# Turns of a constant on TensorE before the first scores, and a part of q moved from GpSimd to VectorE

## The reference

```
scores = q @ k.T / 8
thresh = max(scores) - tau
scores = where(scores >= thresh, scores, -1e9)
attn   = exp(scores - max(scores)); attn = attn / (sum(attn) + 1e-9)
out    = attn @ v
```

## Time and profile before

| | us |
|---|---|
| three runs | 1113.57, 1113.32, 1110.95 |
| median | 1113.32 |
| the profiled execution | 1109.99 |
| its span (first to last instruction) | 1108.2 |

### The profile page before, as it was taken

The page is one execution under the profiler, slowest core; times in us unless marked ns, Lnnn a source line. Parts: engine busy times, 40 slices in busy tenths (PEclk is TensorE's granted clock), DMA queues, the critical chain, the costliest instruction groups (busy, mean ns, idle before and its releaser), DMA issues.

```text
span 1108.2 us, 18294 instructions
## 1 busy us (share of the span) xinstructions
PE 1053.6 (95%) x6504; PEld 988.9 (89%) x6504; DVE 833.9 (75%) x1544; ACT 610.0 (55%) x1121; POOL 513.1 (46%) x594
## 2 busy tenths in 40 slices
PE   4888899999999999998999999989999998999998
PEld 4766799999999999998999999978898988899897
DVE  4999978787878888767885847888584799867561
ACT  4888786868676776644452516445251544534240
POOL 3567755554545564564561405456050546514050
PEclk9999999999999999999999999989999999999999
DMA  4447453437234543462224041432203143330302
GB/s 120 119 135 189 126 136 112 114 94 174 88 110 112 141 112 99 113 167 81 87 87 137 1 134 58 129 97 80 92 1 106 29 124 105 96 124 29 114 1 86
DMA packets 117227, 112.44 MB, mean 101 GB/s; under 512 B 28672, under 2 KB 100496, under 8 KB 117136
## 3 DMA queue, kind: packets, MB, share of 16 engines
q1 hardware_dynamic: 116832, 110.97, 35.6%
q10 hardware_dynamic: 304, 0.30, 0.1%
HBM read 78.12 MB, written 33.10 MB: 100 GB/s over the span
## 4 chain that ended last, share of the span: by engine, by line
PE 79%; DVE 12%; issue 4%; ACT 3%; DMA 1%; POOL 1%; SPq 1%; ACTq 0%; POOLq 0%; DVEq 0%
PE score L785 11%; PE score L824 10%; PE mm L785 8%; PE score L706 8%; PE mm L744 7%; PE tr L721 6%; PE mm L751 6%; PE mm L735 6%; PE tr L824 5%; PE tr L785 4%; PE score L822 3%; DVE prob L927 2%; PE tr L822 2%; PE mm L822 2%; DVE neg_max L919 1%
## 5 line engine op out<-in xcount | busy, mean ns | idle before, releaser
L1593 POOL TENSOR_TENSOR gd_lo<-act_ring,gd_hi 128x384 fp32r<-128x384 f32 x144 | 155.2, 1098 | 289.0 <-ACT gd_hi L1345 287.3
L1236 ACT ACTIVATE pt_hi<-tr 128x640 fp32r<-128x640 f32 x144 | 101.7, 706 | 98.3 <-PE tr L721 97.8
L919 DVE TENSOR_REDUCE neg_max<-score 128x1 f32<-128x576 f32 x144 | 108.3, 752 | 27.4 <-PE score L706 24.5
L945 DVE TENSOR_TENSOR pt_lo<-tr,pt_hi 128x640 fp32r<-128x640 f32 x144 | 118.3, 821 | 10.1 <-ACT pt_hi L1236 9.2
L706 PE MATMUL score<-k_hi,q_sp 128*128 128x288 f32 x320 | 98.3, 323 | 28.8 <-DVE prob L927 20.0
L1536 POOL TENSOR_SCALAR thresh<-neg_max,tau_abs 128x1 f32<-128x1 f32 x144 | 41.7, 290 | 179.3 <-DVE neg_max L919 178.7
L927 DVE SCALAR_TENSOR_TENSOR prob<-score,thresh,prob 128x576 f32<-128x576 f32 x144 | 116.3, 808 | 0.0
L721 PE MATMUL tr<-ident,prob 128*128 128x128 f32 x720 | 105.5, 278 | 8.0 <-issue 5.9
L1231 ACT ACTIVATE prob<-score,neg_max 128x576 f32<-128x576 f32 x144 | 106.5, 739 | 7.8 <-DVE neg_max L919 7.5
L721 PEld LDWEIGHTS tr<-ident,prob 128*128 128x128 f32 x720 | 83.5, 143 | 18.5 <-issue 17.7
L706 PEld LDWEIGHTS score<-k_hi,q_sp 128*128 128x128 f32 x320 | 62.3, 195 | 40.3 <-DVE prob L927 30.2
(11 more groups left out here) (172 smaller groups left out, 3259.1 us busy)
## 6 DMA issues: line engine op xcount, KB each, us to landing
pair_raw<-x_t_scratch SPq DMA_DIRECT2D x72, 192.0 KB, 3.2
q_raw<-in_qT SPq DMA_DIRECT2D x64, 144.0 KB, 2.8
k_raw<-in_kT SPq DMA_DIRECT2D x62, 144.0 KB, 2.9
unit_raw<-in_w_in SPq DMA_DIRECT2D x48, 128.0 KB, 2.5
unit_raw<-in_w_out SPq DMA_DIRECT2D x48, 128.0 KB, 2.3
o_parts_scratch<-o_t SPq DMA_DIRECT2D x32, 160.0 KB, 1.8
x_t_scratch<-x_raw SPq DMA_DIRECT2D x8, 576.0 KB, 3.1
part_t_scratch<-y_out SPq DMA_DIRECT2D x8, 576.0 KB, 3.3
```

Of the source, the lines that this page charges most:

```text
L919: dve.tensor_reduce(neg_max[:, r:r + 1], score[:, g % 2, :, 0:HALF], AX.XY, ALU.max, negate=True).then_inc(max_done, 1)
L945: dve.tensor_tensor(pt_place(pt_lo, x), turned_place(x), pt_place(pt_hi, x), ALU.subtract).then_inc(pt_lo_done, 1)
L1236: act.activation(pt_place(pt_hi, x), turned_place(x), ACT.Copy).then_inc(pt_hi_done, 1)
L1593: pool.tensor_tensor(gd_lo[:, u, c, :], act_ring[:, g % 3, :], gd_hi[:, u, c, :], ALU.subtract).then_inc(g_lo_done, 1)
```

## The change

TensorE runs 32 transposes of `ident` against itself into the bank that the real turns use later, before the first scores. Tile 0 waits for k's high part where it waited for k's low part, and its second matmul waits for the low part. VectorE, not GpSimd, makes the low part of q's first 256 columns, between k's high part and k's low part.

```
@@ tensor: scores(g)
                 if g == 0:
                     pe.wait_ge(first_q_lo_done, 1)
-                    pe.wait_ge(first_k_lo_done, 1)
+                    pe.wait_ge(first_k_hi_done, 1)
...
                     for e, (side, col, k_part) in enumerate(parts):
+                        if g == 0 and half == 0 and e == 1:
+                            pe.wait_ge(first_k_lo_done, 1)
                         m = pe.matmul(score[:, g % 2, half, 0:HALF], q_sp[:, col:col + P],
@@ tensor: start
             pe.wait_ge(consts_done, 8)
+
+            for _ in range(32):
+                pe.transpose(turned_p[:, 0:P], ident[:, :], ident[:, :])
             scores(0)
@@ vector: start
             dve.tensor_copy(k_hi[:, 0, :], k_raw[:, 0, :]).then_inc(first_k_hi_done, 1)
+            begin = slice(0, 2 * P)
+            dve.wait_ge(first_q_scaled, 1)
+            dve.tensor_tensor(q_sp[:, begin], q_raw[:, 0, begin], q_sp[:, begin], ALU.subtract).then_inc(first_q_lo_done, 1)
             dve.wait_ge(first_k_hi_done, 1)
@@ gpsimd: start
-            begin, rest = slice(0, 2 * P), slice(2 * P, S)
-            pool.wait_ge(first_q_scaled, 1)
-            pool.tensor_tensor(q_sp[:, begin], q_raw[:, 0, begin], q_sp[:, begin], ALU.subtract).then_inc(first_q_lo_done, 1)
+            rest = slice(2 * P, S)
             pool.wait_ge(q_scaled, 1)
```

## The result

| | kernel before | changed kernel |
|---|---|---|
| median of 13 runs, us | 1111.17 | 1107.98 |
| lowest and highest, us | 1109.35, 1113.59 | 1106.83, 1112.08 |
| the profiled execution, us | 1109.99 | 1107.62 |

The ratio is 0.9972, with a 95% interval of 0.9961 to 0.9983: 3.1 us faster, between 1.9 and 4.3. That is 0.28%, just inside the 0.3% named above. The median of before came out 2.1 us lower over 13 runs than over the first three. The prediction's range, 1108.0 to 1114.2, was counted from 1113.3: 5.3 us less to 0.9 more. The change of 3.1 us lies inside it, while 1107.98 as a bare time lies at its very edge.

What follows compares the result with a forecast made beforehand. TensorE's work and its waits (79% of the span) were taken to bound the kernel. An earlier first maximum, 0.7, plus one faster tile, 0.5, made 1.2, taken as 1.3 us: 1113.3 to 1112.0 us, range 1108.0 to 1114.2.

Steps and rivals of the forecast that it cites:

- the likeliest case: At the start, TensorE's clock rises with the turns and falls again at about 13 to 14 us; 1112.0 us, chance 0.47.
- The step that decided: TensorE between 9 and 16 us: a stretch emptier than both that ended in falls loses the clock, despite shorter pauses.
- The same: Whole kernel: time stays within 0.3% (3.3 us) of the kernel before; chance 0.67.
- rival A: The clock holds from the start until the dense part; 4.5 us gained, 1108.8 us, chance 0.25.
- the turns: TensorE's 32 opening transposes: start at 1.95, 0.21 us apart, then 0.12; clock rises after 3.4 or 6.8 us of work.
- The subtraction: q's low part on VectorE, 256 columns, behind k's high part: 0.44 us, done at 7.31.
- The first maximum: First row maximum, at 9.65 before: between 0.87 and 0.0 us earlier, taken as 0.7.
- The tiles before the fall: Score tiles run at the high clock before it falls: one tile, 0.5 us, a second in some executions.
- The second rise: The clock's return after its early fall; the forecast sum had no term for it.
- Rival B: The turns don't raise the clock; first score at 8.8 instead of 8.31, 0.5 us lost, 1113.8 us, chance 0.22.
- Rival C: Turns write one tile, so each waits 0.42 us for the last; everything 7.1 us later, 1120.4 us, chance 0.04.
- The two later falls: Clock falls at 507.8 and 726.3 us, worth 1.7 and 2.2 us; a shifted program can lose or gain one.

Runs made afterwards that it cites:

- e3: Changed kernel with further turns of the constant filling TensorE's pauses between the first tiles; 1106.34 us, ratio 0.9958 to the kernel before.
- e1: Changed kernel without the 32 turns; 1109.82 us, ratio 0.9995 to the kernel before.
- e0: Changed kernel again, unedited, for a second profile; 1107.90 us, ratio 0.9980 to the kernel before.
- e10: Changed kernel a third time, unedited, a single execution; 1106.49 us, no ratio.
- e2: Kernel before with the 32 turns alone added; 1108.76 us, ratio 0.9979 to the kernel before.
- e9: Kernel before again, unedited, a single execution for a second profile; 1110.68 us, no ratio.
- e7: Changed kernel with 64 turns instead of 32; 1113.12 us, ratio 1.0017 to the kernel before.
- e8: Changed kernel with fillers in the start's pauses, the quiet pauses behind tiles 15 and 16, and the long pauses between layer parts; 1102.04 us, ratio 0.9917 to before.
- e4: Changed kernel with 16 turns instead of 32; 1109.40 us, ratio 0.9985 to the kernel before.
- e5: e3 plus five more turns in each of the two pauses per pair of heads behind tiles 15 and 16; 1106.30 us, ratio 0.9957 to the kernel before.

## Why the prediction was right, and where it was not

**Right: the likeliest case.** The forecast was that the clock rises with the turns and falls again near 13 to 14 us, and a time within 0.3%. The traces show the rise at 7.0 (6.2 and 7.7 in the others), the fall at 13.8 (13.0, 14.5), and 0.28%. The step that decided, that a stretch emptier than both that ended in a fall would not keep the clock although its pauses are shorter, held in all three traces, and e3 shows the other side of it. As a rule it is weaker than that: the fall of e3 at 52.7 and the pause of 2.79 us with and without a fall don't follow it.

**Partly luck: the class.** "The same" was forecast from a gain of 1.3 us and came with one of 3.1, 0.2 us short of the 0.3%. The range held 3.1 only because it was drawn down to rival A, which did not happen.

**Right: the turns.** First at 1.97, 0.21 us apart, then 0.12; the rise came 5.0 us after the first, between the 3.4 and 6.8 of the prediction. The subtraction took 0.43 us for 0.44 forecast. The split wait did what it says (e1).

**Wrong in size: the sum.** It was 0.7 + 0.5 = 1.2, taken as 1.3; the change is worth 3.1. The terms, by the first profile:

- *The first maximum* was put at 0.7 earlier; it came 0.97 earlier. The working had 0.87 for turns that don't delay, and 0.7 was a cut for turns that might. They hardly did: the second matmul started at 8.07 where 8.2 was reckoned, as k's low part was done at 7.83 and not at 8.11. In e0, where the rise came last of the three, it was 0.63, in e10 0.98.
- *The tiles before the fall* were put at one, 0.5 us. Tile 2 to tile 3 took 2.39 instead of 2.92, which is that 0.53; the tile in which the fall stands saved another 0.22. In e0, with the fall at 14.5, tiles 2 and 3 both ran in 2.4.
- *The second rise* was taken to come after the same work as before. In e2 it came at 20.4 and in e10 partly at 19.8, which puts the ninth tile at 29.24 and 29.49. I had no term for that.

Together the start gave 1.8 to 2.5 us in three traces. The rest, up to 3.1, lies behind it. From the ninth tile to the last matmul before took 1073.1 and 1073.7 us, the change 1072.6, 1072.7 and 1072.0: about 1 us on the mean. These traces don't show it to be the change's. In the first trace of before VectorE's pause that ends at 725.86 lasted 3.03 us; in the change, timeline of PE, it is shorter:

```profile
723.64 0.54 PE L787 MATMUL mm<-xs_hi,ws_hi 128*128 128x384 f32 x1 [2.39 <-DVE y_ring L1065]
```

That is 0.64 us, but e9, the kernel before itself, has 2.51 there, and what e9 loses is 1.0 us at its longer fall near 505. **The baseline** was the other error: 1112.0 was worked out from the median of three runs, which was 2.1 us over that of 13.

**Rival A** (the clock holds) fell in every trace of the change. Its price was near: it had 3.7 us for the clock held to the ninth tile, and e3, which holds it, measures 31.87 - 26.89 = 4.98 in all, of which 0.94 is the earlier first maximum, so 4.0. The rule of the Trainium skill, "TensorE: Matmul & The Clock Gate", table "Why this matters for your kernels", that pauses matter when they are long, does not cover this case: the fall came with pauses of 1.96 and 1.58 us. The section "A second HAM failure mode: psum-queue depth-cycling" of the same page of the Trainium skill, that frequent short pauses make the clock swing, agrees with it.

**Rival B** (the turns don't raise the clock) fell: the rise came among turns alone, with no other matmul yet issued, in every trace with 32 or 64 of them. Trace of the change, line L841 (ns shortest/median/longest, first and last start):

```profile
L841 PE MATMUL tr<-ident x32: 272/421/477, 2.0 to 7.8; 128*128 128x128 f32 x32
```

Both levels stand in one line of turns, 421 and 272 ns. The sentence of the Trainium skill, same page, "Part 4: PE-mode transpose", that the full clock does not engage for transpose-mode, does not hold for these turns, neither for their speed nor for their counting as activity. The trace calls them MATMUL; that `pe.transpose` is the mode which that page means is taken from its name.

**Rival C** (0.42 us per turn, since they write one place) fell by the same trace: 32 in 6.13 us. The price of a late start was right: e7 delays the first score by 3.4 us and the ninth tile by as much.

**The two later falls** were priced at 1.7 and 2.2 us. The second price is too high: four of its 15 matmuls run before a pause of 2.13 us that VectorE ends at 729.88, so they delay nothing, and 11 x 0.15 = 1.6 is the better estimate. e8 removes both falls and the one near 52 us, about 1, for 0.0041 of the time against e3 (4.5 us). The parts can't be told apart by these intervals, but the size is that of the sum, 4.3.

## What to carry to other kernels

Raising TensorE's clock before the first real matmul pays only as far as the work behind it keeps the clock; look at how busy TensorE will be between its first bursts and how long it will pause, and fill those pauses with work that nobody waits for, of a length that ends before the wait does. Take each place in the trace where matmuls of one shape change their duration, read the stretch before it, and price it: here the filler at the start, at two quiet tiles and at the joints was worth 0.6% on top of the change, 0.83% with it, where the change alone gave 0.2 to 0.3%. Keep the opening turns as short as raising the clock allows, because everything behind them waits.

## What the runs showed of the hardware that was not expected

- Turns of a constant (128x128 float32) raise the clock by themselves; the rise came 2.9 to 5.7 us after the first one in nine traces. 16 of them, ending at 5.4 us, raised nothing in the one trace of e4, though the mean clocks of its other runs suggest that they sometimes do.
- The same work gets the rise in one execution and not in another: eight scores and five turns, unbroken, in e2 and e4 but not in either trace of before. The same idle time of 2.8 us brings a fall in e5 and e7 and none in before or in the change.
- A fall can follow a stretch as dense as one that kept the clock: 5.25 us busy of 7 before the fall at 52.7 in e3, 5.37 of 7 from 9 to 16 us without one.
- With no fall left, the scatter between runs shrank from 5.6 us (11 runs) to 1.2 (6).
